# Leaving out the filler products of the attention rounds that have no early expert products

## The reference

```
for t in range(S):
    y[:, :, t] = einsum('bhd,bhde->bhe', q[:, :, t], state)
    v_old = einsum('bhde,bhd->bhe', state, kt)
    state = state + bt * einsum('bhd,bhe->bhde', kt, vt - v_old)
```

## Time and profile before

| | us |
|---|---|
| median of 3 runs | 2386.44 |
| lowest and highest | 2384.58, 2386.55 |
| profiled execution, own time | 2386.57 |
| its span, first to last instruction | 2384.8 |
| mean granted TensorE clock of the span | 0.997 |

### The profile page before, as it was taken

How to read it: one execution, slowest core, us unless ns; L and a number is a source line. 1 busy time by engine, 2 the same in 40 slices (tenths; PEclk the granted TensorE clock), 3 DMA queues, 4 the chain that set the end, 5 groups by cost and what they waited for, 6 DMA issues and landing times.

```text
span 2384.8 us, 35935 instructions
## 1 busy us (share of the span) xinstructions
PE 2342.4 (98%) x14643; PEld 1939.5 (81%) x14643; DVE 1020.1 (43%) x2003; ACT 641.9 (27%) x1207; POOL 1168.4 (49%) x1043
## 2 busy tenths in 40 slices
PE   5999999999999999999999999999999999999999
PEld 4888888888778888888888888888888888888887
DVE  5977676664433333333343333333433432322222
ACT  3444444444321111111111111111111223223222
POOL 4555454442165454454555555455545575444432
PEclk9999999999999999999999999999999999999999
DMA  3133333232322121221221222122211210000001
GB/s 105 58 117 125 109 113 112 98 114 90 125 77 64 50 50 36 56 71 60 50 83 51 65 66 84 49 49 84 80 51 51 83 41 14 27 14 14 14 23 58
DMA packets 124916, 159.95 MB, mean 67 GB/s; under 512 B 6672, under 2 KB 72656, under 8 KB 124752
## 3 DMA queue, kind: packets, MB, share of 16 engines
q1 hardware_dynamic: 124752, 157.65, 21.5%
HBM read 122.40 MB, written 35.23 MB: 66 GB/s over the span
## 4 chain that ended last, share of the span: by engine, by line
PE 74%; DMA 0%; DVE 0%; ACT 0%; issue 0%; SPq 0%; DVEq 0%
PE bank L1385 41%; PE bank L1370 31%; PE bank L210 2%; DMA w_raw<-route_dram 0%; DMA route_dram<-x_sum 0%; PE bank L1307 0%; PE bank L1392 0%; PE bank L1299 0%; ACT L1444 0%; ACT h_out L220 0%; DVE route L1561 0%; DVE rowsum L1555 0%; DVE rowsum L1559 0%; DVE route L1573 0%; DVE colsum L1565 0%
## 5 line engine op out<-in xcount | busy, mean ns | idle before, releaser
L1260 POOL TENSOR_TENSOR h_hl<-h_out,h_hl 128x512 fp32r<-128x512 f32 x480 | 617.8, 1294 | 832.2 <-ACT h_hl L1461 832.2
L1385 PE MATMUL bank<-h_hl,w_hl 128*128 128x512 f32 x4320 | 994.1, 389 | 0.4 <-issue 0.4
L1385 PEld LDWEIGHTS bank<-h_hl,w_hl 128*128 128x128 f32 x4320 | 810.8, 188 | 169.0 <-issue 0.7
L1461 ACT CAST h_hl<-h_out 128x512 fp32r<-128x512 f32 x480 | 296.3, 620 | 1100.4 <-DVE h_out L1522 1081.6
L1370 PE MATMUL bank<-x_early,w_hl 128*128 128x512 f32 x1836 | 427.2, 391 | 5.6 <-DVE h_out L1522 5.1
L1370 PEld LDWEIGHTS bank<-x_early,w_hl 128*128 128x128 f32 x1836 | 346.3, 189 | 78.4 <-DVE h_out L1522 5.5
L1522 DVE SCALAR_TENSOR_TENSOR h_out<-bank,w_raw 128x512 f32<-128x512 f32 x268 | 185.3, 692 | 374.0 <-PE bank L1370 348.7
L1370 PE MATMUL bank<-x_late,w_hl 128*128 128x512 f32 x1440 | 332.9, 389 | 0.0
L1370 PEld LDWEIGHTS bank<-x_late,w_hl 128*128 128x128 f32 x1440 | 270.3, 188 | 56.1
L1543 DVE TENSOR_TENSOR x_sum<-x_sum,bank 128x512 f32<-128x512 f32 x216 | 146.9, 686 | 348.7 <-PE bank L1385 348.7
L210 PE MATMUL bank<-x_early,w_hl 128*128 128x512 f32 x1044 | 281.6, 406 | 0.0
(11 more groups left out here) (118 smaller groups left out, 1709.4 us busy)
## 6 DMA issues: line engine op xcount, KB each, us to landing
w_raw<-in_moe_w SPq DMA_DIRECT2D x48, 768.0 KB, 5.2
h_early<-h_out SPq DMA_DIRECT2D x116, 256.0 KB, 2.0
h_raw<-h_early SPq DMA_DIRECT2D x29, 1024.0 KB, 5.4
w_raw<-route_dram SPq DMA_DIRECT2D x96, 256.0 KB, 4.9
kq_t<-in_kq_rows SPq DMA_DIRECT2D x48, 256.0 KB, 2.8
kv<-in_kv_cols SPq DMA_DIRECT2D x24, 384.0 KB, 3.3
w_raw<-in_moe_w_in SPq DMA_DIRECT2D x4, 768.0 KB, 4.4
w_raw<-in_moe_w_out SPq DMA_DIRECT2D x4, 768.0 KB, 5.0
```

The lines of the kernel that those rows point to most:

```text
L1260: pool.tensor_tensor(h_hl[:, s % 2, 1, f, :], gated[:, n % 2, :], h_hl[:, s % 2, 0, f, :].bitcast(F32), ALU.subtract).then_inc(pool_lo, 1)
L1385: m = pe.matmul(bank[:, 4 + kc, :], w2_hl[hn % 2][:, a, f, kc * P:(kc + 1) * P], h_hl[:, s % 2, c, f, :], start=n + f == 0, stop=n == len( ...
L1461: act.copy(h_hl[:, s % 2, 0, f, :], gated[:, n % 2, :]).then_inc(act_h, 1)
```

## The change

The constant and the loop that issues the fillers go. In rounds -1 to 4 `early` now does nothing. That takes away 7 x 4 matmuls in each of six rounds, 168 in all, with their weight loads. All other instructions of all engines, their order and their waits stay as they are.

```diff
@@ -63,7 +63,6 @@
 EARLY_FROM = 5
 UPS = 5
-BUSY = 4
@@ -546,10 +545,6 @@
                         def early(first, end):
 
                             if not EARLY_FROM <= p < PAIRS:
-                                if -1 <= p < EARLY_FROM and first < 4 * PRODUCTS:
-                                    for _ in range(BUSY):
-                                        pe.matmul(bank[:, BE + 1, 3 * P:4 * P], ident16[:, :], ident16[:, :],
-                                                  start=True, stop=True)
                                 return
```

## The result

Without the fillers the kernel takes 2393.84 us, the median of 9 runs (2390.24 to 2395.66). The kernel before took 2386.44 us beside it (9 runs, 2384.01 to 2388.2). That is 7.4 us slower, a ratio of 1.003 with a 95% interval of 1.0021 to 1.0039.

A forecast was written before the change was run, and what follows sets the result against it. TensorE was taken to bound the kernel, with VectorE bounding much of each early round. Three falls at 1.25 us, two rounds at -0.21 and round -1's +1.0 less 0.2 give +4.1 us: 2390.5 us, range 2385 to 2397.

The forecast's parts named there:

- my own case: Rounds 0 to 4: the clock falls in some of them, 2387.5 to 2393 us; chance 0.48.
- rival (b): Rounds 0 to 4: the clock falls in every round, 2393.5 us, or 2403 with long low stretches; chance 0.27.
- my own signs of being wrong: Clock 1.00 throughout rounds 0 to 4, a fall starting in or outlasting the dense part, or later stages absorbing the shift.
- the longer price: Low clock lasting through and beyond the dense part, where TensorE sets the pace: 6.8 us low, up to +2.9 us a fall.
- What the fillers cost: Rounds 0 to 4: removing them gains 0.21 us a round, TensorE's excess that VectorE waits for at the dense part's end.
- Where the clock falls: Rounds 0 to 4: at the end of the thin part, where TensorE waits for VectorE's masks, in some rounds.
- My yardstick: Weight-load time left in round 1's thin part, 1.38 us, against 1.39 us ahead of the fall in the kernel before.
- Rival (a): Rounds 0 to 4: the clock holds without fillers, 2385.7 us; chance 0.22.
- How many falls: Rounds 0 to 4: three of the five rounds chosen to have a fall of the clock.
- The price of a fall: Dense part of a round: 3.4 us low at 0.5 us per us, less 0.46 of fillers: +1.25 us, bounds +0.4 to +2.9.
- Round -1: The clock falls earlier there: +1.0 us, between 0 and +3, less 0.2 us of fillers.
- Carried to the end: Rounds -1 to 4 feed a TensorE stage without slack: round 5 about 4 us later, the rest moved by the same.

The follow-up runs named there:

- e3_thin_only: Kernel before, fillers of rounds -1 to 4 kept only where TensorE waits for VectorE's masks (120 of 168): 2383.22 us, ratio 0.999.
- e5_dense_only: Kernel before, fillers of rounds -1 to 4 kept only where TensorE sets the pace (48 of 168): 2397.16 us, ratio 1.0039, 5 runs.
- e4_narrow: Kernel before, all 168 fillers kept with their weight loads, each streaming 8 columns in place of 128: 2391.43 us, ratio 1.0023.
- e7_thin_two: Kernel before, fillers kept only in rounds -1 and 0, there only where TensorE waits for masks (40 of 168): 2390.12 us, ratio 1.0018.
- e2_last_four: Kernel before, fillers kept in rounds 1 to 4 and left out in rounds -1 and 0: 2390.23 us, ratio 1.0019.
- e6_round_m1: Kernel before, fillers kept in round -1 alone: 2392.9 us, ratio 1.0028, 6 runs.

## Why the prediction was right, and where its sum was wrong

The forecast said slower, 2390.5 us in a range of 2385 to 2397, for the reason that the clock falls in some of the rounds. It was slower for that reason, by 7.4 us and not 4.1. The time lies just above the 2387.5 to 2393 that I gave to my own case and is nearly that of rival (b), but not by its mechanism: the clock did not fall in every round. One of my own signs of being wrong came true: the low stretch lasted through the dense part, the longer price.

**What the fillers cost.** Taken as 0.21 us a round. Round 2 of the profiled execution has no low stretch and is 0.24 us shorter than before (17.48 against 17.72). Round 3 is 0.27 us longer: there the subtraction (line 808 before, 803 now) took 0.88 us in place of 0.36, and 0.51 less 0.24 is that 0.27. This term was right, and a source of 0.5 us either way in a round was missing beside it.

Before:

```profile
99.52 0.36 DVE L808 TENSOR_TENSOR rhs_hl<-rhs,rhs_hl 128x192 bf16<-128x192 f32 x1
```

In the changed kernel:

```profile
108.59 0.88 DVE L803 TENSOR_TENSOR rhs_hl<-rhs,rhs_hl 128x192 bf16<-128x192 f32 x1
```

**Where the clock falls.** Right: behind the thin part, in some rounds. e3_thin_only against e5_dense_only shows that the fillers of the thin part decide, and e4_narrow that their streamed columns do, and not the queue. My yardstick was a poor one, though: I compared the time of weight loads that would be left with that ahead of the one fall, and in e4_narrow all of them were left and the clock fell. Rival (a), that it holds, is out. By the Trainium skill, "TensorE: Matmul & The Clock Gate", section "Why this matters for your kernels", what keeps the clock up is to leave no long idle gaps between bursts; the falls in rounds 0 to 2 came with no wait of TensorE above 1.3 us in the 10 us ahead of them, so the measurement decides against reading it that way.

**How many falls.** I took three, in rounds 0 to 4; the profiled execution has two, in rounds 0 and 1. The two groups of e7_thin_two, with their mean clocks, say that the count differs between executions of one program.

**The price of a fall.** This is the step that failed, with the sentence "in the dense part it is full from the first, so I take half of that, 3.4 us". The low stretch lasted 10.2 us, longer than even the 6.8 us that I took as its upper end, and did so in all eight profiled falls behind a thin part of rounds 0 to 2 (in the changed kernel, e2_last_four, e4_narrow, e5_dense_only, e6_round_m1 and e7_thin_two). A busy row of TensorE had misled me: busy for 10.00 of 10.00 us, it was not brought back up. That this is because the dense part consists mostly of products of 48 or 64 columns behind weight loads of 128, with one group of grams of 256, is argued from e4_narrow and not shown by itself. The price, 3.7 us in round 1 of the changed kernel and 4.2 in round 2 of e7_thin_two (21.66 against 17.48), is 0.36 to 0.41 us per us at the low clock, between the 0.25 and 0.5 that I had as bounds. With 3.7 in place of 1.25 for each of two rounds with a fall, -0.21 for each of the other three and the measured +1.9 of round -1, the sum is +8.7 us; the profiled execution is 8.6 us longer. (What line 808 added in round 3 and what the wait behind 660 us gave back, below, cancel in part.) With three falls at that price, as I had counted, it would have been about +12.6 us, or 2399 us, outside my range. So one fall too many and a price too low made up for each other in part, and that the time fell into the range is in that respect luck.

**Round -1.** Taken as +1.0 less 0.2, for an earlier fall; measured +1.9. The clock did not fall earlier, it had not come up: it rose at 47 us and not at 28. The missing fillers don't always have that effect: e2_last_four has none in round -1 either, and there the clock rose at 29.3 us, fell at 32.7 and was back at 46.4. Either way most of round -1 passed at the low clock. That was a part of the cost that I weighed too lightly, though it lay in the range.

**Carried to the end.** Right: 9.2 us late at round 5, 9.5 at 651 us, 8.6 in the span. The 0.8 us in between is the shorter wait at 660 us, within the 1 to 2 us either way that I gave it.

What stays open: why a thin part brings a fall and an equal one does not, in one execution or in two of one program. Who wins the tie of line 808 fits as a condition (no fall in 9 where VectorE won, three in 12 where it lost). The start of a thin part relative to the moments at which the clock changes fits as the other. Neither was varied by itself.

## What to carry to other kernels

Put fillers first where TensorE waits for another engine; where it sets the pace they cost their time and here did least. Then price a missing one not by its own time but by the low stretch behind it, here 10 us at about 0.4 us per us. A full busy row is no sign that the clock will come back: look at what streams in it. When a kernel's runs form two groups, look for a clock that changes in only some of them, and judge a variant by its range and not by one profile.

## What the runs showed of the hardware

- In rounds 0 to 2 the clock fell from 2.4 to 1.2 GHz behind stretches in which TensorE never waited more than 1.3 us (43 matmuls in 3.4 us), and stayed low for 10.2 us with TensorE busy for 10.0 of 10.0 us.
- Two thin parts of one execution with 43 matmuls in 3.4 us and a wait of 1.27 and 1.28 us each: the clock fell behind the first and not behind the second.
- With 168 matmuls of 8 columns the clock fell in round 0 as without them (2391.43 us); with 168 of 128 columns and the same weight loads it had no fall there (2385.78 us).
- VectorE's subtraction of 128 x 192 takes 0.36 or 0.88 us and GpSimd's product beside it 0.90 or 0.67, for the same two instructions, started in the same hundredth of a microsecond.
- One program gave 2385.1 to 2387.2 us in five runs, with a mean granted clock of 0.996 or 0.997, and 2389.9 to 2395.9 in seven, with 0.992 to 0.995, on one chip.
